# A fused attention and two-layer MLP kernel: another add releases the first product of each quad, and the last stores leave from two queues

## The reference

```
s = kn.transpose(0, 2, 1) @ qn / tau          # kn, qn: k and q over their column norms
a = softmax(s)
x = v @ a
...
h = x @ w_in;   g = h - tanh(h);                              x = g @ w_out       # MLP 1, 2048 hidden
...
h = x @ w_in2;  g = where(h > 0, h, exp(min(h, 0)) - 1);      y = g @ w_out2      # MLP 2, 2048 hidden
```

## Time and profile before

| | us |
|---|---|
| three runs | 1082.26, 1082.47, 1084.25 (median 1082.47) |
| the profiled execution, its own time | 1082.65 |
| its span, from first to last instruction | 1080.9 |
| PE busy (modelled ends) | 1041.3, 96% of the span |
| DVE busy | 824.8, 76% |
| ACT busy | 758.5, 70% |
| mean granted clock of PE | 0.993 of 2.4 GHz |

### The profile page before, as it was taken

One profiled execution on the slowest core, in us unless ns is written; L12 is line 12 of the kernel. 1 busy time (PEld: TensorE's weight loads), 2 busy tenths in 40 slices (PEclk: granted clock), 3 DMA queues, 4 the chain that ended last, 5 costly groups with the idle time before them and its releaser, 6 DMA issues.

```text
span 1080.9 us, 13685 instructions
## 1 busy us (share of the span) xinstructions
PE 1041.3 (96%) x4556; PEld 854.6 (79%) x4556; DVE 824.8 (76%) x1378; ACT 758.5 (70%) x1340; POOL 0.8 (0%) x7
## 2 busy tenths in 40 slices
PE   8979999999999999999999999999999999999996
PEld 7847778888888888888787887887887887888895
DVE  5758987777776876775898887787787787787765
ACT  6556776766766766766668776877777786777773
POOL 0000000000000000000000000000000000000000
PEclk9999999999999999999999999999999999999999
DMA  9912002102102001012113003003002101100201
GB/s 358 301 31 39 1 1 58 21 1 62 17 1 59 15 1 40 1 39 69 48 51 103 1 1 79 0 1 73 7 1 60 20 1 47 28 1 0 39 2 34
DMA packets 117558, 46.24 MB, mean 43 GB/s; under 512 B 100336, under 2 KB 108528, under 8 KB 117232
## 3 DMA queue, kind: packets, MB, share of 16 engines
q1 hardware_dynamic: 117056, 44.45, 15.4%
q10 hardware_dynamic: 432, 0.92, 0.3%
HBM read 33.03 MB, written 12.32 MB: 42 GB/s over the span
## 4 chain that ended last, share of the span: by engine, by line
PE 85%; DVE 8%; issue 3%; ACT 2%; DMA 1%; SPq 0%; ACTq 0%; DVEq 0%
PE r_ps L282 14%; PE r_ps L284 14%; PE r_ps L283 14%; PE x_ps L282 6%; PE x_ps L284 5%; PE x_ps L283 5%; PE z_ps L282 3%; PE z_ps L284 3%; PE z_ps L283 3%; PE x_ps L289 2%; PE q_ps L289 2%; PE q_ps L282 2%; PE q_ps L283 2%; PE q_ps L284 2%; PE y_ps L284 2%
## 5 line engine op out<-in xcount | busy, mean ns | idle before, releaser
L515 ACT ACTIVATE g_hi<-g 128x512 fp32r<-128x512 f32 (+1 forms) x384 | 236.8, 617 | 172.1 <-DVE g L720 74.3
L591 DVE TENSOR_TENSOR g_lo<-g,g_hi 128x512 fp32r<-128x512 f32 (+1 forms) x384 | 259.4, 676 | 51.6 <-ACT g_hi L515 43.1
L282 PE MATMUL r_ps<-g_hi,w_out_hi 128*128 128x512 f32 (+1 forms) x768 | 297.1, 387 | 0.4 <-DVE g_lo L591 0.4
L283 PE MATMUL r_ps<-g_lo,w_out_hi 128*128 128x512 f32 (+1 forms) x768 | 296.6, 386 | 0.0
L284 PE MATMUL r_ps<-g_hi,w_out_lo 128*128 128x512 f32 (+1 forms) x768 | 296.5, 386 | 0.0
L282 PEld LDWEIGHTS r_ps<-g_hi,w_out_hi 128*128 128x128 f32 x768 | 144.7, 188 | 28.3 <-DVE g_lo L591 0.8
L284 PEld LDWEIGHTS r_ps<-g_hi,w_out_lo 128*128 128x128 f32 x768 | 144.6, 188 | 27.5
L283 PEld LDWEIGHTS r_ps<-g_lo,w_out_hi 128*128 128x128 f32 x768 | 144.8, 189 | 27.2
L282 PE MATMUL x_ps<-t_hi,w_ops 128*128 128x512 f32 (+1 forms) x288 | 117.8, 409 | 20.2 <-DVE w_ops L591 12.7
L284 PE MATMUL x_ps<-t_hi,w_ops 128*128 128x512 f32 (+1 forms) x288 | 111.5, 387 | 0.0
L283 PE MATMUL x_ps<-t_lo,w_ops 128*128 128x512 f32 (+1 forms) x288 | 111.4, 387 | 0.0
(11 more groups left out here) (106 smaller groups left out, 1496.8 us busy)
## 6 DMA issues: line engine op xcount, KB each, us to landing
v_blocks<-v_dram SPq DMA_DIRECT2D x40, 128.0 KB, 3.0
x_scratch<-side SPq DMA_DIRECT2D x20, 256.0 KB, 2.1
vt<-x_scratch SPq DMA_DIRECT2D x20, 256.0 KB, 3.6
out_dram<-side SPq DMA_DIRECT2D x80, 64.0 KB, 1.9
k_ring<-k_dram SPq DMA_DIRECT2D x9, 512.0 KB, 8.5
q_ring<-q_dram SPq DMA_DIRECT2D x9, 512.0 KB, 9.3
w_in_sb<-moe_w_in_dram SPq DMA_DIRECT2D x1, 2048.0 KB, 9.5
w_out_raw<-moe_w_out_dram SPq DMA_DIRECT2D x1, 2048.0 KB, 15.2
```

The costliest lines, as they stand in the source:

```text
L282: nc.tensor.matmul(ps, w_hi, m_hi, start=start, stop=False, skip_group_check=True)
L283: nc.tensor.matmul(ps, w_hi, m_lo, start=False, stop=False, skip_group_check=True)
L515: nc.scalar.activation(g_hi[b][n % DEPTH[b]][:, 0:width], g[b][:, 0:width], ACT.Copy).then_inc(g_rounded[b], 1)
L591: return nc.vector.tensor_tensor(lo, x, hi.bitcast(F32), ALU.subtract)
```

## The change

Four edits. First, `P1` of quad n waits for `h_ready["12"]` of the quad before (the add L797 that reads bank X), where it waited for `g_ready["12"]` (the form_g 12 made from the sum, four to six DVE instructions later). Second, in the last quad alone, `P4` is issued ahead of `second(n - 1, "12")`. Third, after the last quad, the block 12 of g is multiplied before block 21 (the order was the reverse), and the last four transposes run with j = 1 first. Fourth, the 16 stores of the last pair are split: SP issues those of every other block of 32 partitions, ACT the others.

```diff
+        def out_part(p, m, j, b):
+            n, channel = WIDTH[p], m * P + b * BLOCK
+            rows = out[TOKEN0[p] + j * n:TOKEN0[p] + (j + 1) * n, :].rearrange("(e i) c -> i e c", i=BLOCK)
+            return (rows[:, :, channel:channel + BLOCK],
+                    side[b * BLOCK:(b + 1) * BLOCK, m, j, 0:n].rearrange("i (e c) -> i e c", c=BLOCK))
...
-            store_out(PAIRS - 1)
+            for j in (1, 0):
+                for m in range(CC):
+                    sp.wait_ge(r_moved[j], CC * 2 * PAIRS - CC + m + 1)
+                    for b in range(0, P // BLOCK, 2):
+                        to, source = out_part(PAIRS - 1, m, j, b)
+                        sp.dma_start(to, source).then_inc(out_stored, 16)
...
-                order = ("11", "22", "21", "12") if n % QUADS == 0 else ("11", "22", "12", "21")
+                order = ("11", "22", "21", "12") if n % QUADS == 0 and n < ALL else ("11", "22", "12", "21")
...
-                wait(pe, g_ready["12"], n)
+                wait(pe, h_ready["12"], n)
                 product(n, P1, X, True).then_inc(p1_done, 1)
...
-                between(n, 2)
+                if n < ALL - 1:
+                    between(n, 2)
                 pe.wait_ge(h_ready["22"], n + 1)
                 product(n, P4, Z, False).then_inc(h_ready["21"], 1)
+                if n == ALL - 1:
+                    between(n, 2)
                 between(n, 3)
...
             round_g(ALL - 1, "21")
+            for j in (1, 0):
+                for m in range(CC):
+                    act.wait_ge(r_moved[j], CC * 2 * PAIRS - CC + m + 1)
+                    for b in range(1, P // BLOCK, 2):
+                        to, source = out_part(PAIRS - 1, m, j, b)
+                        act.dma_start(to, source).then_inc(out_stored, 16)
...
             split_g(ALL - 1, "21")
-            for j in range(2):
+            for j in (1, 0):
                 for m in range(CC):
                     turn_out(PAIRS - 1, m, j)
```

More of the change, by code:

```diff
@@ L237, in store_out @@
             def store_out(p):
-                n = WIDTH[p]
                 for j in range(2):
-                    rows = out[TOKEN0[p] + j * n:TOKEN0[p] + (j + 1) * n, :].rearrange("(e i) c -> i e c", i=BLOCK)
                     for m in range(CC):
@@ L243, in store_out @@
                         for b in range(P // BLOCK):
[L244 to L247, removed]
+                            to, source = out_part(p, m, j, b)
+                            sp.dma_start(to, source).then_inc(out_stored, 16)
             for p in range(PAIRS - 1):
```

## The result

| | before | changed |
|---|---|---|
| median of 4 runs, us | 1082.74 | 1070.75 |
| lowest and highest, us | 1082.26, 1084.25 | 1069.57, 1071.45 |
| profiled execution, own time / span, us | 1082.65 / 1080.9 | 1069.57 / 1067.8 |

The ratio is 0.9886 with a 95% interval of 0.9869 to 0.9903. The forecast was 1070.1 us.

A forecast was written before the change was run, and what follows sets the result against it. PE was taken as the bound, in the second half kept waiting at P1 for form_g 12. Savings of 9.5 + 0.3 + 2.6 = 12.4 us took 1082.65 to 1070.25, as a median 1070.1 us; 8-in-10 range 1067.0 to 1074.5.

The forecast's parts named there:

- Ordinary quads: Second half: each quad regains the 0.17 us lost at P1, 5.7 us for 34; six of 448 columns give 0.9 us.
- The slack at P6: P6's wait for the copy of X to Y: 0.36 us free, 0.19 us left at the faster pace.
- Quads with u = 1: Five quads after transposes: 0.32 us each, 1.6 us in all; about 1 us of each stall moves to P6 and second 22.
- Between the halves: Quads 42 to 50, where DVE is full: 1.3 us in all, bounds 0.5 and 3 us.
- the one for quads 47 and 48: P4 of quad 47 comes earlier and the small wait at P1 of quad 48 goes: 0.35 us together.
- The last quad: P4 ahead costs 0.35 us, the new block order returns 0.65 us: net 0.3 us, bounds −0.35 and 0.65.
- The stores: The last 16 stores from two queues take 5.6 us instead of 8.2: 2.6 us saved, bounds 0 and 4.1.
- no gain on the stores: Rival at the last stores: both queues feed through one descriptor path; 9.8 us gained in all, 1072.7 us. Chance 0.17.
- the wait moving to P6 in every quad: Rival: the loop over ACT is longer than read, 40 quads gain nothing; 5.8 us in all, 1076.7. Chance 0.08.
- a slower clock: Rival: PE's granted clock falls, about 1.5 us a fall, nine more needed to eat 12.4 us. Chance 0.02.
- the case with more gain: Rival: stores give 4.1 us and the stretch between the halves 3; 15.6 us in all, 1066.9. Chance 0.14.
- starts anew: Claim that the DVE and ACT chain restarts from P7 and P3 each quad, so 0.17 us does not add up.

The follow-up runs named there:

- e1: The kernel before with only P1's wait changed from form_g 12 to the add L797: 1074.42 us, ratio 0.9923.
- e11: The changed kernel with three one-column activations ahead of the copy of X to Y on ACT, quads 51 to 95: 1073.08 us, ratio 0.9907.
- e10: The changed kernel with one one-column activation ahead of the copy of X to Y on ACT, quads 51 to 95: 1070.8 us, ratio 0.9888.
- e4: The changed kernel with the two transposes of j = 0 moved behind form_g 22 in quad u = 0: 1068.05 us, ratio 0.9865.
- e9: e4 plus the j = 1 transposes between form_g 21 and split_g 12 and the last quad's P4 in its old place: 1065.16 us, ratio 0.9834.
- e2: The changed kernel with P1's old wait for form_g 12, so only the changes at the end: 1079.72 us, ratio 0.9973.
- e7: The changed kernel with the copy of X to Y put behind the round of 21 on ACT: 1105.59 us, ratio 1.0207.
- e3: The changed kernel with P4 of the last quad back behind second(94, 12): one run of 1070.4 us.
- e6: The changed kernel with all 16 last stores on SP again, in the new block order: 1073.76 us, ratio 0.9913.
- e5: e4 plus the two transposes of j = 1 put ahead of form_g 21 in quad u = 1: 1066.65 us, ratio 0.9848.

## Why the prediction was right

- **Ordinary quads**, 5.7 us forecast for 34 and 0.9 for the six of 448 columns: 5.50 and 1.01. e1 shows that the one line does it. The slack at P6 that lets the gain through was forecast as 0.19 us left; 0.26 us are left (0.31 less a signal of 0.05). I had doubled ACT's signal out of caution; e11 and quad 57 show 0.05 us, as for DVE. e10 shows that there is slack, e11 that 0.28 us use it up.
- **Quads with u = 1**, 1.6 us forecast, 1.15 measured. The mechanism was right: of the 1.35 us of each stall about 1.1 moved to P6 and second 22, and e4 and e9 take it away at those two places. The mis-sized term is the delay from the transposes' end to the load, 0.12 us instead of 0.05, and the fifth quad, with 448 columns, gave 0.13 us where I took it like the others (10.41 us against 10.54; the other four gave 0.25 or 0.26 each), and why it gave less was not tried.
- **Between the halves**, 1.3 us forecast, 1.08 measured, with 0.8 us of scatter. Distances of P7 divide it. From quad 42 to 47 they give 51.97 and 51.85 us with the old wait (before and e2) and 51.19 to 51.31 with the new one (e7 left out here): 0.5 to 0.8 us, where I took 0.5; whether by shorter waits of DVE on ACT, as I had it, was not tried. From 49 to 50 it is 11.14 and 11.18 against 10.64 to 10.69: 0.45 to 0.54 us, forecast 0.45. The step that failed is the one for quads 47 and 48, 0.35 us forecast: from P7 of 47 to P7 of 48 it is 9.67 and 9.75 with the old wait, 9.75 to 10.30 with the new one, so nothing or a loss. P4 of quad 47, which I had coming earlier, now waits for h22 (timeline of PEld). The 0.8 us of scatter lie in this distance and in that from 40 to 42. DVE stays the bound there: PE's wait for h22 grew from 4.7 to 6.9 us in all, as the wait at P1 went. The second row is from the changed kernel's view of waits (us in total, times, longest):

```profile
566.71 0.19 PEld L291 LDWEIGHTS z_ps<-t_hi,w_ops 128*128 128x128 f32 x1 [0.65 <-DVE h L814]
```

```profile
PE z_ps L291 <- DVE h L814: 6.9, 6, 2.5
```

- **The last quad**, 0.3 us forecast, 0.45 measured, of which some 0.1 us is not the change's. The matmuls of 448 columns behind P7 of quad 95 follow each other at 0.2065 us in some profiled executions (before, e2, e4, e10) and at 0.203 in the others, also where the code of this stretch is the same: e4 and e10 take 9.44 and 9.45 us for it, the changed kernel 9.30. At like distances the two edits give 0.31 us (before against e2) and 0.38 (e1 against changed), which is the forecast. P4 ahead costs 0.36 us (forecast 0.35), and the order of the blocks gives 0.74 (e1 against e3; forecast 0.65). Why two distances occur is open.
- **The stores**, 2.6 us forecast, 2.70 measured, but the step was in part wrong. I held the engines to a share of 1.0 as the ceiling, 5.3 us of work. The share went to 1.43 in a window of 4 us, and to 1.06 over the whole of the issuing. What kept the saving from the 4.1 us of halved issuing was the landing, 2.5 to 2.7 us instead of 1.8, and a tail of pieces behind the last issue: issuing ended at 1064.85, the kernel 2.95 us later, where it was 1.8 us before. The Trainium skill ("DMA: Bandwidth & Descriptors", section "Issuing engines are not separate DMA queues") says that a second issuer saves only issuing time; the trace agrees, in that the 2.7 us saved lie within the 4.1 us of issuing that went. Its "usually small" does not hold for these stores: 8.16 us of issuing for 0.9 MB, and e6 shows 2.7 us of it come back with a second queue. The page's rule speaks of shared DMA engines, not of one descriptor path as my rival did; each queue kept its pace, 0.52 and 0.53 us a store.
- **The rivals**: no gain on the stores, refuted by e6; the wait moving to P6 in every quad, refuted by the ordinary quads; e7 shows what it would have cost had the copy stood one round later; a slower clock, not seen (0.993 both times). Of the case with more gain, the stores gave 2.70 us and not 4.1, the stretch between the halves 1.08 and not 3.
- **What I stated and the runs corrected**: that the chain of DVE and ACT "starts anew" in each quad. Here it did where no engine's list was late. In e5 a delay of 1.2 us in quad 57 shows as 0.27 us in quad 58.

## What to carry to other kernels

When one late wait is removed, read the slack of the next waits in the engine's own order before counting the gain: here 0.17 us a quad went through 0.46 us of slack whole, while a stall of 1.35 us came back at the next two waits but for 0.25. The cause of this stall was four transposes that stood early in another engine's list; moving them (e9) took another 5.3 us off the five quads, where the change of the wait had taken 1.15. A wait for the last reader of a buffer is enough where the buffer is only overwritten.

## What the runs showed of the hardware

- A weight load that comes late in a stream of matmuls costs its lateness less about 0.08 us: 0.25 us late costs 0.17 (before), 0.23 costs 0.15 (e11, quad 61), 0.74 costs 0.66 (e7). Loads 0.11 us late went with 0 to 0.03 us more (e11, quads 60 and 52).
- From the recorded end of what a load waits for to the load it is 0.05 us behind a form_g of DVE or a copy of ACT and 0.12 us behind the transposes of DVE.
- An activation of one column is recorded with 0.19 us but takes 0.09 us in ACT's stream, and three take 0.28, so its recorded length overstates what it delays.
- Two queues that issue at the same time keep the pace of one: 0.52 and 0.53 us a store against 0.51.
- The DMA share of the window view passes 1: 1.43 with two queues of 128-byte pieces, against 0.62 to 0.65 with one.
